# Attention by head pairs and query parts, the last queries of two heads in one tile, and the first MLP begun inside the first batch

## The chip, the cores and the metric

The kernel runs on one core of a Trainium2 chip. The metric is the device time of one execution in microseconds; the smaller the better. The core has TensorE (matmuls and transposes into the PSUM banks), VectorE, ScalarE, GpSimd and SyncE, each with its own queue of instructions worked off in order; they wait for each other by semaphores. In the profile they are PE (PEld for the loads of its stationary operand), DVE, ACT, POOL and SP.

## The reference

Three stages, all in float32 with an accuracy that the kernel reaches by splitting each matmul operand in a high and a low part and taking three products (or two, where one side needs no low part).

```python
def _attn_ref(q, k, v, s):                     # 4 batches, 8 heads, 576 tokens, 64 per head
    scores = scale * np.matmul(q, k.transpose(0, 1, 3, 2))
    cum = np.cumsum(np.maximum(s, 0.0), axis=-1)
    bias = -(cum[:, :, :, None] - cum[:, :, None, :])
    scores = np.where(causal, -1000000000.0, scores + np.minimum(bias, 0.0))
    attn = np.exp(scores - np.max(scores, axis=-1, keepdims=True))
    attn = attn / (np.sum(attn, axis=-1, keepdims=True) + 1e-09)
    return np.matmul(attn, v)

def _moe_ref(x, w_in, w_out, g_ln):            # 2304 tokens, 512 -> 1024 -> 512
    h = x @ w_in
    solu = h * softmax(h)
    ln = (solu - mean) / np.sqrt(var + 1e-06) * g_ln
    return ln @ w_out

def _moe2_ref(x, w_in, w_out):                 # 512 -> 2048 -> 512
    h = x @ w_in
    return (h * np.clip(h + 3.0, 0.0, 6.0) / 6.0) @ w_out
```

## The kernel before

One loop over slots `n` is written out for every engine; all engines run through the same slots and meet by counting semaphores. A head has five slots (`SLOTS`), one for each tile of 128 queries; the fifth tile has 64 (`TAIL`). In slot `k` of head `m` TensorE transposes the block row `k` of head `m`'s exponentials (`transpose_probs`, L488), and computes scores of head `m + 1` (`scores`, L474 to L478): four to five slots ahead of their transposes. VectorE adds the bias and takes the row maximum (`row_max`, L678), ScalarE the exponential and its row sum (`exp_row`, L835). The transposed block is copied by ScalarE as its high part (`copy_probs`, L846) and subtracted by VectorE for the low one (`split_probs`, L689). `weighted_values` (L507) multiplies with v for the queries of `CUTS`: the first 256 and the other 320; hi and lo of v stand side by side, so a product comes in two halves of partitions that `copy_corr` (ScalarE, L854) and `add_parts` (VectorE, L705) add into `xT`. For a pair of heads `scales` (L522) transposes the widened reciprocals of the sums and `scale_pair` (L713) multiplies.

SyncE loads q and k of a head together (each half of the 128 partitions gets the same 64 rows), its bias row and v. ScalarE rounds q and k (`split_qk`, L827), GpSimd subtracts the low part of q in the upper 64 partitions (L385) and of k (L387), splits v (L395, L397), widens the reciprocals (L402) and splits `w_in` in 16 parts (L409, L411).

The first MLP works on 18 tiles of 128 tokens (`t`), ten slots each (`TILE_SLOTS`), from slot `MOE_FROM` = 45 on, behind nine heads. Of a tile, `hidden` (L538) takes six slots, four matmuls each; then VectorE takes the maximum (`max1`), ScalarE the exponential (`exp1`, L871), VectorE the normalised product (`solu`, L729 to L737), ScalarE the square (`square`), GpSimd the reciprocal root, VectorE `norm` (L742). In the next tile's slots come the transposes (`transpose_ln`, L553) with copy and split, and `project` (L572): the tile pair's projection to 256 tokens, two of the four column blocks a tile, into one PSUM bank that ScalarE empties (`copy_x2`, L889). Two buffers `es` hold the exponentials of two tiles. From tile 12 (`ALONE`) there is no attention left, and hidden tiles take turns in two pairs of banks.

The attention of a batch must be complete before a token tile that lies in it is read: `split_x` waits for `x_done`. SyncE loads the first six chunks of the second MLP's weights when attention has ended, GpSimd splits them in the last five tiles' slots (`split_early`), and the second MLP follows, six groups of three token tiles, 16 chunks each (`hidden2`, L592 to L594, and `output`, L609 to L611). The order on TensorE is this loop:

```python
for n in range(-SLOTS, MOE_TO):
    m, k = n // SLOTS, n % SLOTS
    t, r = (n - MOE_FROM) // TILE_SLOTS, (n - MOE_FROM) % TILE_SLOTS
```

## Time and profile before

| | |
|---|---|
| device time, median of 2 runs | 961.86 us (961.58 to 962.13) |
| the profiled execution | 965.07 us, its span 963.0 us |
| TensorE busy | 866.0 us, 90% of the span |
| VectorE, ScalarE, GpSimd busy | 425.9, 435.1, 253.5 us |
| mean granted clock of TensorE | 0.958 of full speed |
| DMA | 51.38 MB |

The span goes from the first to the last instruction of the profile; the device time has about 2 us more. Busy is the time in which at least one instruction of the engine runs; a matmul's end is modelled, and matmuls overlap, so their mean length is more than the distance between their starts. Full speed of TensorE is 2.4 GHz, the other level 1.2 GHz.

### The profile page before, as it was taken

The page shows a single profiled execution, that of the slowest core. Times are in us where ns is not written, and L with a number is a line of the kernel's source. Part 1 is how long each engine was busy: PE and PEld are TensorE (multiplying, and loading weights), DVE is VectorE, ACT ScalarE, POOL GpSimd, SP SyncE. Part 2 cuts the span into 40 slices and gives each one's busy share as a digit, 9 for nine tenths or more (in the row PEclk, how much of TensorE's full clock was granted, in tenths as well). Part 3 has the DMA queues.
Part 4 walks back from the last instruction along what each step waited for, and adds up shares of the span by engine and source line. Part 5 has one row for each costly group of instructions (what it writes and reads, how often), then busy time and mean ns, then how long its engine had stood idle before and what let it go on. Part 6 is the DMA issues. An engine that isn't in the chain of part 4 may idle for free.

```text
span 963.0 us, 13828 instructions
## 1 busy us (share of the span) xinstructions
PE 866.0 (90%) x5008; PEld 765.0 (79%) x5008; DVE 425.9 (44%) x1037; ACT 435.1 (45%) x985; POOL 253.5 (26%) x291
## 2 busy tenths in 40 slices
PE   4588868988889989888988999999999999999997
PEld 3467647777777877776877999999999999999996
DVE  3466565666666666664434412233222222232222
ACT  4577665666666676663323335322222222222222
POOL 4477433443433443421364025100000000000000
PEclk9788778799999999999999999999999999999999
DMA  6554313313223322203000203000000000000000
GB/s 153 171 173 122 99 44 87 82 49 87 68 62 88 86 62 69 54 16 132 1 1 1 88 19 114 1 33 0 28 6 1 33 1 1 34 1 1 33 1 34
DMA packets 25779, 51.38 MB, mean 53 GB/s; under 512 B 5424, under 2 KB 9520, under 8 KB 25712
## 3 DMA queue, kind: packets, MB, share of 16 engines
q1 hardware_dynamic: 25712, 50.50, 18.3%
q8 instruction: 41, 0.67, 0.3%
q14 instruction: 26, 0.21, 0.1%
HBM read 45.69 MB, written 4.79 MB: 52 GB/s over the span
## 4 chain that ended last, share of the span: by engine, by line
PE 65%; ACT 12%; DVE 9%; issue 6%; POOL 4%; DMA 3%; SPq 1%; ACTq 0%; DVEq 0%; POOLq 0%
PE psum L538 9%; PE psum L594 7%; PE psum L592 7%; PE psum L610 7%; PE psum L593 7%; PE psum L611 7%; PE psum L609 7%; PE psum L572 4%; PE psum L507 4%; ACT prob L835 4%; PE psum L488 3%; DVE es L733 2%; ACT psum L877 2%; ACT qk_st L827 2%; DVE nmax L724 2%
## 5 line engine op out<-in xcount | busy, mean ns | idle before, releaser
L791 DVE SCALAR_TENSOR_TENSOR act<-act,psum 128x384 f32<-128x384 f32 x96 | 53.2, 554 | 292.0 <-ACT act L939 292.0
L939 ACT ACTIVATE act<-psum,three 128x384 f32<-128x384 f32 x96 | 55.8, 581 | 274.8 <-PE psum L594 274.8
L594 PE MATMUL psum<-x_hi,w_lo 128*128 128x384 f32 x384 | 129.5, 337 | 0.0
L592 PE MATMUL psum<-x_hi,w_hi 128*128 128x384 f32 x384 | 129.4, 337 | 0.0
L593 PE MATMUL psum<-x_lo,w_hi 128*128 128x384 f32 x384 | 129.0, 336 | 0.0
L835 ACT ACTIVATE prob<-prob,nmax 128x128 f32<-128x128 f32 (+4 forms) x160 | 95.8, 601 | 56.1 <-DVE nmax L678 55.2
L611 PE MATMUL psum<-w_hi,g_lo 128*128 128x512 f32 x288 | 113.9, 395 | 0.0
L610 PE MATMUL psum<-w_lo,g_hi 128*128 128x512 f32 x288 | 113.7, 395 | 0.0
L609 PE MATMUL psum<-w_hi,g_hi 128*128 128x512 f32 x288 | 112.0, 389 | 0.0
L488 PE MATMUL psum<-ident,prob 128*128 128x128 f32 (+1 forms) x480 | 78.6, 275 | 34.7 <-DVE pB_lo L689 16.9
L488 PEld LDWEIGHTS psum<-ident,prob 128*128 128x128 f32 (+1 forms) x480 | 54.1, 147 | 54.9 <-issue 38.4
L474 PE MATMUL psum<-qk_st 128*128 128x128 f32 (+2 forms) x192 | 76.7, 404 | 20.1 <-POOL k_lo L387 12.8
L572 PE MATMUL psum<-lnT_hi,w_out_hi 128*128 128x256 f32 x288 | 82.2, 286 | 13.6 <-ACT xT L889 13.4
L678 DVE CUSTOM_DVE_ANT_0 prob<-psum,bias 128x128 f32<-128x128 f32 (+4 forms) x160 | 83.2, 535 | 10.8 <-DMA bias<-cum_dram 8.3
L572 PE MATMUL psum<-lnT_lo,w_out_hi 128*128 128x256 f32 x288 | 82.1, 285 | 0.0
L572 PE MATMUL psum<-lnT_hi,w_out_lo 128*128 128x256 f32 x288 | 81.6, 283 | 0.0
L478 PE MATMUL psum<-k_lo,qk_st 128*128 128x128 f32 (+2 forms) x192 | 78.3, 408 | 0.0
L592 PEld LDWEIGHTS psum<-x_hi,w_hi 128*128 128x128 f32 x384 | 72.2, 188 | 4.1
L593 PEld LDWEIGHTS psum<-x_lo,w_hi 128*128 128x128 f32 x384 | 72.1, 188 | 4.0
L538 PE MATMUL psum<-w_in_hi,xs_hi 128*128 128x512 f32 x144 | 62.3, 432 | 12.9 <-POOL xs_lo L422 12.9
L594 PEld LDWEIGHTS psum<-x_hi,w_lo 128*128 128x128 f32 x384 | 72.0, 188 | 0.0
L689 DVE TENSOR_TENSOR pB_lo<-psum,pB_hi 128x384 fp32r<-128x384 f32 (+2 forms) x96 | 55.4, 577 | 33.9 <-ACT pB_hi L846 33.9
(92 smaller groups left out, 1834.4 us busy)
## 6 DMA issues: line engine op xcount, KB each, us to landing
qk_raw<-qkT SPq DMA_DIRECT2D x64, 288.0 KB, 4.2
bias<-cum_dram SPq DMA_DIRECT2D x32, 288.0 KB, 4.0
out<-out_sb SPq DMA_DIRECT2D x6, 768.0 KB, 3.5
v_raw<-v_main SPq DMA_DIRECT2D x32, 128.0 KB, 3.5
w_raw<-w_in SPq DMA_DIRECT2D x16, 256.0 KB, 3.3
w_raw<-w_out SPq DMA_DIRECT2D x16, 256.0 KB, 3.9
w_in_raw<-w_in SPq DMA_DIRECT2D x1, 2048.0 KB, 9.4
w_out_raw<-w_out SPq DMA_DIRECT2D x1, 2048.0 KB, 9.8
```

The costliest lines, as they stand in the source:

```text
L478: last = pe.matmul(ps, q, k_lo[p][:, lo_:hi_], start=False, stop=True)
L488: last = pe.transpose(ps[:, j * w:(j + 1) * w], prob[0:w, src:src + P], ident[0:w, 0:w])
L538: last = pe.matmul(bank(h_bank(t) + half), x, w, start=(n % 12 == 0), stop=(n % 12 == 11))
L572: last = pe.matmul(bank(project_bank(q), PJW), w, x, start=(n == 0), stop=(n == 23))
L592: pe.matmul(ps, w2_hi[f][:, cols], xh, start=(c_ == 0), stop=False)
L593: pe.matmul(ps, w2_hi[f][:, cols], xl, start=False, stop=False)
L594: last = pe.matmul(ps, w2_lo[f][:, cols], xh, start=False, stop=(c_ == NC - 1))
L609: pe.matmul(bank(4 + k), gh, w2_hi[f][:, NC * P:], start=(f == 0), stop=False)
L610: pe.matmul(bank(4 + k), gh, w2_lo[f][:, NC * P:], start=False, stop=False)
L611: last = pe.matmul(bank(4 + k), gl, w2_hi[f][:, NC * P:], start=False, stop=(f == NF2 - 1))
L678: dve.tensor_tensor_reduce(out=prob[0:rows, BLK[i] * P:BLK[i] * P + n], in0=psum[0:rows, at:at + n], in1=bias[p][0:rows, 0:n], scale=-SCAL ...
L835: sc.activation(tile, tile, ACT.Exp, scale=-1.0, bias=nmax[0:rows, p, i:i + 1], accum_out=rsum[0:rows, p, i:i + 1]).then_inc(exp_done, 1)
```

## The change

**Units.** A unit is a head pair and a part of the queries. The first kind has the first 256 queries (tiles 0 and 1), two items: item `k` has both tiles of head `k`. The second kind has the other 320, five items: tile 2 and tile 3 of head 0, the same of head 1, and as fifth item the last 64 queries of both heads in one tile of 128 rows. For that tile q of one head stands in columns 0 to 63 and of the other in 64 to 127, with zeros in the rest, and the scores of both heads are added in one bank. A batch is four units of the first kind and then four of the second: 28 items, 112 in all, instead of 160 slots. q and k of a head are loaded and split twice, for its first unit (256 and 256 columns) and for its second (384 and 576), into three buffers; v too (two blocks, then five). The sums of a pair are scaled once a unit.

**Distance.** Scores run two items ahead of their transposes, in three banks; the fifth block of an item 4 is transposed into a free piece of bank 2, and the scores of a later item that need the bank of an item 4 wait for that item's `split_probs`.

**The first MLP** begins at item 14. A tile `t` has six steps, laid on the items `STARTS[t]` to `STARTS[t + 1]`, 9, 9, then 7 and 6 items long; 14 tiles begin and the loop ends at item 134. Hidden and projection matmuls stand ahead of and behind the scores of the item. There is one buffer `es`, one pair of hidden banks (but for tile 16) and one bank for projections and the transposes of the MLP. `split_x`'s high part and `copy_x2` move from ScalarE to VectorE, where `max1` and `solu` stand ahead of the item's row maximum. `w_in` is loaded in four DMAs from item 0 on and split from item 3 on, `w_out` is split at items 24 to 31. The early chunks of the second MLP load behind the last scaling and are split at items 120 to 131.

```diff
+PAIRS = HEADS // 2
+UNITS = BATCH * 2 * PAIRS
+FIRST_KIND = [u % (2 * PAIRS) < PAIRS for u in range(UNITS)]
+BASE = [0]
+for _kind in FIRST_KIND:
+    BASE.append(BASE[-1] + (2 if _kind else 5))
+ITEMS = BASE[UNITS]
+ITEM = [(u, k) for u in range(UNITS) for k in range(BASE[u + 1] - BASE[u])]
+TILES = [((0, k, k), (1, k, 2 + k)) if FIRST_KIND[u] else
+         ((2 + k % 2, k // 2, 2 * (k % 2) + k // 2),) if k < 4 else ((4, None, 4),) for u, k in ITEM]
+TILES_BEFORE = [0]
+LOS_BEFORE = [0]
+for _tiles in TILES:
+    TILES_BEFORE.append(TILES_BEFORE[-1] + len(_tiles))
+    LOS_BEFORE.append(LOS_BEFORE[-1] + (2 if _tiles[0][0] == NQ - 1 else 1))
+S_BANKS = [((2 * (u % PAIRS) + k) % 3,) if FIRST_KIND[u] else ((0,), (1,), (2,), (0,), (1, 2))[k] for u, k in ITEM]
+S_BEFORE = [max([m for m in range(n) if set(S_BANKS[m]) & set(S_BANKS[n])], default=-1) for n in range(ITEMS)]
+TAIL_AT = 2 * BANK - 288
...
+STARTS = [14, 23] + [32 + 7 * i for i in range(4)] + [60 + 6 * i for i in range(8)] + [109, 116, 122, 128, 134]
+STEPS = 6
+END = STARTS[NT]
+STEP_AT = {}
+for _t in range(NT):
+    for _r in range(STEPS):
+        STEP_AT[STARTS[_t] + _r * (STARTS[_t + 1] - STARTS[_t]) // STEPS] = (_t, _r)
+FIRST_STEP = STARTS[0]
 W_IN_PARTS = 16
+W_IN_FROM, W_OUT_FROM, EARLY_FROM = 3, 24, 120
...
+def sums_slot(u, e):
+    return BASE[u + 1] + (1 if FIRST_KIND[u] else e)
+def scales_slot(u):
+    return BASE[u + 1] + 2
...
+SPLIT_AT = {}
+for _u in range(UNITS):
+    SPLIT_AT.setdefault(BASE[_u] - 3, []).append((_u, 0))
+    SPLIT_AT.setdefault(BASE[_u] - (2 if FIRST_KIND[_u] and _u % (2 * PAIRS) else 1 if _u else 2), []).append((_u, 1))
+VALUES_SLOT = {}
+VALUES_AT = {}
+for _u in range(UNITS):
+    for _e in range(2):
+        VALUES_SLOT[_u, _e] = BASE[_u] + (1 + _e if not FIRST_KIND[_u] else _e)
+        VALUES_AT.setdefault(VALUES_SLOT[_u, _e], []).append((_u, _e))
+X_AT = {STARTS[t] - 2: t for t in range(NT)}
...
-        es = [sb(first, f"es{p}", [P, F1]) for p in range(2)]
+        es = sb(first, "es", [P, F1])
...
+            def scores(n):
+                u, k = ITEM[n]
+                c = kind(u)
+                last_load = load_of(u, 1 if k == 4 else TILES[n][0][1])
+                pe.wait_ge(q_lo_done, last_load + 1)
+                pe.wait_ge(k_lo_done, last_load + 1)
+                if S_BEFORE[n] >= 0:
+                    pe.wait_ge(max_done, TILES_BEFORE[S_BEFORE[n] + 1])
+                    if ITEM[S_BEFORE[n]][1] == 4:
+                        pe.wait_ge(pT_lo_done, LOS_BEFORE[S_BEFORE[n] + 1])
+                    elif 2 in S_BANKS[n] and any(ITEM[m][1] == 4 for m in range(max(0, n - 5), n)):
+                        m = max(m for m in range(n) if ITEM[m][1] == 4)
+                        pe.wait_ge(pT_lo_done, LOS_BEFORE[m + 1])
+                for tile, e, _ in TILES[n]:
+                    at, w = scores_of(n, tile), KW[tile]
+                    q_at = (tile if c else tile - 2) * P
+                    diag0 = tile * P
+                    heads = (0, 1) if e is None else (e,)
+                    for lo_, hi_ in [(0, w)] if w <= BANK else [(0, w // 2), (w // 2, w)]:
                         ps = psum[:, at + lo_:at + hi_]
-                        pe.matmul(ps, q, k_hi[:, lo_:hi_], start=True, stop=False)
-                        if hi_ > diag0:
-                            pe.matmul(psum[:, at + diag0:at + hi_], ident_bf[:, :], mask_bf[:, 0:hi_ - diag0],
-                                      start=False, stop=False)
-                        last = pe.matmul(ps, q, k_lo[p][:, lo_:hi_], start=False, stop=True)
+                        for e_ in heads:
+                            p = load_of(u, e_) % 3
+                            q = qk_hi[p][:, q_at:q_at + P]
+                            keys = slice(QW[c] + lo_, QW[c] + hi_)
+                            pe.matmul(ps, q, qk_hi[p][:, keys], start=(e_ == heads[0]), stop=False)
+                            if hi_ > diag0 and e_ == heads[0]:
+                                mask = mask_tail if e is None else mask_bf
+                                pe.matmul(psum[:, at + diag0:at + hi_], ident_bf[:, :], mask[:, 0:hi_ - diag0],
+                                          start=False, stop=False)
+                            last = pe.matmul(ps, q, qk_lo[p][:, keys], start=False, stop=(e_ == heads[-1]))
                 last.then_inc(scores_ready, 1)
 
-            def transpose_probs(m, i):
-                pe.wait_ge(exp_done, NQ * m + i + 1)
-                n = SLOTS * m + i
-                wait(pe, pT_lo_done, n if n >= MOE_FROM else n - 1)
-                ps, w = bank(turn(m, i)), ROWS[i]
-                for j in range(i + 1):
-                    src = (BLK[i] + j) * P
-                    last = pe.transpose(ps[:, j * w:(j + 1) * w], prob[0:w, src:src + P], ident[0:w, 0:w])
...
+            def transpose_probs(n):
+                pe.wait_ge(exp_done, TILES_BEFORE[n + 1])
+                before = n - 2 if n <= FIRST_STEP else n - 1
+                if before >= 0:
+                    pe.wait_ge(pT_lo_done, LOS_BEFORE[before + 1])
+                ps = bank(turn(n))
+                j = 0
+                for tile, _, _ in TILES[n]:
+                    for b in range(tile + 1):
+                        src = prob_of(n, tile) + b * P
+                        dst = psum[:, FIFTH:FIFTH + P] if b == NQ - 1 else ps[:, j * P:(j + 1) * P]
+                        last = pe.transpose(dst, prob[:, src:src + P], ident[:, :])
+                        j += 1
                 last.then_inc(pT_ready, 1)
 
-            def weighted_values(h, c):
-                pe.wait_ge(v_lo_done, h + 1)
-                pe.wait_ge(pT_lo_done, NQ * h + (2, NQ)[c])
-                if c == 1:
-                    pe.wait_ge(sum_done, 2 * h + 1)
-                elif h % 2 == 0:
...
+            for n in range(-2, END):
+                t, r = STEP_AT.get(n, (None, None))
+                if n in SCALES_AT:
+                    scales(SCALES_AT[n])
+                for u, e in SUMS_AT.get(n, ()):
+                    weighted_values(u, e)
+                if 0 <= n < ITEMS:
+                    transpose_probs(n)
+                if r in (1, 2) and t >= 1:
+                    transpose_ln(t - 1, r - 1)
+                if r in (0, 1, 2):
+                    hidden(t, 8 * r, 8 * r + (8, 4, 4)[r])
+                if r in (3, 4, 5) and t >= 2:
+                    q = 2 * (t - 2) + (r - 3) // 2
+                    project(q, (0, 16, 8)[r - 3], (8, 24, 16)[r - 3])
+                if 0 <= n + 2 < ITEMS:
+                    scores(n + 2)
+                if r in (1, 2):
+                    hidden(t, 8 * r + 4, 8 * r + 8)
+                if r in (3, 4, 5) and t >= 2:
+                    q = 2 * (t - 2) + (r - 2) // 2
+                    project(q, (8, 0, 16)[r - 3], (16, 8, 24)[r - 3])
 
             for g in range(NG):
...
+            def split_x(t):
+                dve.wait_ge(x_done, units_before(t))
+                wait(dve, h_ready, t)
+                dve.tensor_copy(xs_hi[:, :, :], xT[:, :, t * P:(t + 1) * P]).then_inc(xs_hi_done, 1)
...
+            def copy_x2(q):
+                g, d = q // NC, q % NC
+                dve.wait_ge(x2_ready, q + 1)
+                dve.tensor_copy(xT[:, d, PJW * g:PJW * (g + 1)], bank(L_BANK, PJW)).then_inc(x2_done, 1)
...
+            for n in range(-2, END + 1):
+                t, r = STEP_AT.get(n, (None, None))
+                if r == 0 and t >= 3:
+                    copy_x2(2 * (t - 3) + 1)
+                if r == 3:
+                    max1(t)
+                if r == 4:
+                    solu(t)
+                if 0 <= n + 1 < ITEMS:
+                    for tile, e, col in TILES[n + 1]:
+                        row_max(n + 1, tile, e, col)
+                for u, e in SUMS_AT.get(n, ()):
+                    add_parts(u, e)
+                if 0 <= n < ITEMS:
+                    split_probs(n)
+                for u in range(UNITS):
+                    if BASE[u + 1] == n:
+                        invert(u)
+                if n in SCALES_AT:
+                    scale_pair(SCALES_AT[n])
+                if n in X_AT:
+                    split_x(X_AT[n])
+                if r == 0 and t >= 1:
+                    norm(t - 1)
+                if r in (1, 2) and t >= 1:
+                    split_ln(t - 1, r - 1)
+                if r == 4 and t >= 2:
+                    copy_x2(2 * (t - 2))
+                if W_OUT_FROM <= n < W_OUT_FROM + NF1:
+                    split_w_out(n - W_OUT_FROM)
+                if t == NT - 1 and r in (1, 2, 4, 5):
+                    split_x2(0, (1, 2, 4, 5).index(r))
+            norm(NT - 1)
+            copy_x2(NPJ - NC - 1)
...
+            behind = consts_done, 4
+            w_in_next = 0
+            for n in range(-3, END + 1):
+                t, r = STEP_AT.get(n, (None, None))
+                if n + 1 in STARTS[:NT]:
+                    behind = split_x(STARTS.index(n + 1))
+                if r == 5:
+                    behind = variance(t)
+                for u in range(UNITS):
+                    if BASE[u + 1] == n:
+                        behind = widen(u)
+                for u, e in VALUES_AT.get(n, ()):
+                    behind = split_v(u, e)
+                for u, e in SPLIT_AT.get(n, ()):
+                    behind = split_qk(u, e, behind)
+                for _ in range(1 if n < 8 else 2):
+                    if n >= W_IN_FROM and w_in_next < W_IN_PARTS:
+                        behind = split_w_in(w_in_next)
+                        w_in_next += 1
+                if n >= EARLY_FROM and n - EARLY_FROM < 2 * EARLY:
+                    split_early(n - EARLY_FROM)
...
+            for n in range(-3, END):
+                t, r = STEP_AT.get(n, (None, None))
+                sums = n in SUMS_AT
+                if 0 <= n < ITEMS and not sums:
+                    copy_probs(n)
+                if 0 <= n + 1 < ITEMS:
+                    for i, (tile, e, col) in enumerate(TILES[n + 1]):
+                        exp_row(n + 1, i, tile, col)
+                for u, e in SUMS_AT.get(n, ()):
+                    copy_corr(u, e)
+                if 0 <= n < ITEMS and sums:
+                    copy_probs(n)
+                if r in (1, 2) and t >= 1:
+                    copy_ln(t - 1, r - 1)
+                if r == 3:
+                    exp1(t)
+                if r == 4:
+                    square(t)
+                if W_OUT_FROM <= n < W_OUT_FROM + NF1:
+                    split_w_out(n - W_OUT_FROM)
+                if t == NT - 1 and r in (1, 2, 4, 5):
+                    split_x2(0, (1, 2, 4, 5).index(r))
+                for u, e in SPLIT_AT.get(n, ()):
+                    split_qk(u, e)
...
+    tails = np.zeros((NH, DH, P), np.float32)
+    tails[0::2, :, :TAIL] = qT[0::2, :, cut:]
+    tails[1::2, :, P - TAIL:] = qT[1::2, :, cut:]
     arrays = {
-        "qkT": np.stack([x.reshape(NH, SEQ, DH).transpose(0, 2, 1) for x in (q, k)], axis=2),
-        "v_main": v[:, :cut].reshape(NH, NQ - 1, P, DH).transpose(0, 2, 1, 3).reshape(NH, P, (NQ - 1) * DH),
+        "qk0": np.concatenate([qT[:, :, :CUT], kT[:, :, :CUT]], axis=2),
+        "qk1": np.concatenate([qT[:, :, CUT:cut], tails, kT], axis=2),
+        "v_main": v[:, :cut].reshape(NH, NQ - 1, P, DH).transpose(0, 2, 1, 3),
         "v_tail": v[:, cut:],
         "s": s.reshape(NH, SEQ),
```

`hidden`, `project`, `max1`, `exp1`, `solu`, `square`, `variance`, `norm`, `copy_ln`, `split_ln` and the second MLP keep their arithmetic.

## Rows read from the trace of the kernel before

**Rows 1.** Table of windows: stretch, its length, busy us (instructions) by engine, clock, DMA
```profile
...
0.00:113.00 113.00, 76.89 (x452) 65.41 (x453) 60.45 (x194) 70.37 (x177) 67.14 (x95) 0.84 0.53 147
113.00:189.00 76.00, 61.48 (x314) 50.01 (x315) 48.42 (x123) 46.60 (x108) 28.70 (x31) 0.77 0.25 65
189.00:441.50 252.50, 225.56 (x1574) 195.40 (x1573) 160.49 (x432) 162.65 (x397) 97.18 (x111) 1.00 0.24 65
441.50:543.50 102.00, 87.55 (x551) 77.79 (x552) 42.60 (x68) 32.47 (x64) 35.75 (x42) 0.97 0.14 46
543.50:963.00 419.50, 414.55 (x2122) 376.34 (x2121) 113.91 (x221) 123.04 (x244) 24.70 (x12) 1.00 0.06 21
```

**Rows 2.** Timeline of TensorE: starts of five hidden tiles (start us, us, instruction)
```profile
...
113.00 0.77 PE L538 MATMUL psum<-w_in_hi,xs_hi 128*128 128x512 f32 x1 [0.30 <-POOL xs_lo L422]
...
206.32 0.47 PE L538 MATMUL psum<-w_in_hi,xs_hi 128*128 128x512 f32 x1
...
433.48 0.47 PE L538 MATMUL psum<-w_in_hi,xs_hi 128*128 128x512 f32 x1
...
455.14 0.50 PE L538 MATMUL psum<-w_in_hi,xs_hi 128*128 128x512 f32 x1 [1.33 <-POOL xs_lo L422]
...
529.26 0.50 PE L538 MATMUL psum<-w_in_hi,xs_hi 128*128 128x512 f32 x1 [2.10 <-POOL xs_lo L422]
```

**Rows 3.** List of waits of TensorE over the span
```profile
...
PE psum L488 <- DVE pB_lo L689: 16.9, 18, 4.0
PE psum L488 <- ACT prob L835: 16.2, 22, 2.0
PE psum L572 <- ACT xT L889: 13.4, 10, 2.4
```

**Rows 4.** Groups of instructions by form, GpSimd: count, busy us, mean ns, idle before
```profile
...
L387 POOL TENSOR_TENSOR k_lo<-qk_raw,qk_st 128x576 fp32r<-128x576 f32 x32 | 45.6, 1426 | 2.5
...
L397 POOL TENSOR_TENSOR v_sp<-v_raw,v_sp 128x320 fp32r<-128x320 f32 x32 | 27.9, 872 | 2.6
...
L395 POOL CAST v_sp<-v_raw 128x320 fp32r<-128x320 f32 x32 | 19.0, 595 | 0.0
...
L411 POOL TENSOR_TENSOR w_in_lo<-w_in_raw,w_in_hi 128x256 fp32r<-128x256 f32 x16 | 11.7, 731 | 1.3
...
L409 POOL CAST w_in_hi<-w_in_raw 128x256 fp32r<-128x256 f32 x16 | 6.3, 397 | 10.5 <-DMA w_in_raw<-w_in 10.5
```

**Rows 5.** The same view, VectorE and ScalarE on attention's blocks
```profile
...
L689 DVE TENSOR_TENSOR pB_lo<-psum,pB_hi 128x512 fp32r<-128x512 f32 x32 | 22.0, 687 | 10.5 <-ACT pB_hi L846 10.5
...
L846 ACT ACTIVATE pB_hi<-psum 128x512 fp32r<-128x512 f32 x32 | 18.8, 588 | 1.0 <-PE psum L488 1.0
```

**Rows 6.** Timeline from 396.8 to 401.6 us
```profile
...
396.84 0.36 PE L572 MATMUL psum<-lnT_hi,w_out_hi 128*128 128x256 f32 x1 [1.22 <-ACT xT L889]
...
397.87 0.60 PE L488 MATMUL psum<-ident,prob 128*128 128x128 f32 x4
397.98 0.14 DVE L729 TENSOR_SCALAR den<-esum 128x1 f32<-128x1 f32 x1
...
398.22 0.47 PE L474 MATMUL psum<-qk_st 128*128 128x512 f32 x1
...
399.68 0.15 DVE L737 TENSOR_SCALAR neg_mu<-solu_sum 128x1 f32<-128x1 f32 x1
...
401.12 0.49 PE L488 MATMUL psum<-ident,prob 64*128 64x64 f32 x5 [0.66 <-ACT prob L835]
```

**Rows 7.** Timeline from 136.9 to 142.2 us
```profile
...
136.90 0.75 DVE L717 SCALAR_TENSOR_TENSOR w_out_lo<-w_out_raw,g_sb,w_out_hi 128x512 fp32r<-128x512 f32 x1 [1.88 <-ACT w_out_hi L860]
...
140.17 1.42 POOL L385 TENSOR_TENSOR qk_st<-qk_raw,qk_st 64x576 fp32r<-64x576 f32 x1 [4.74 <-ACT qk_st L827]
...
140.76 1.37 DVE L717 SCALAR_TENSOR_TENSOR w_out_lo<-w_out_raw,g_sb,w_out_hi 128x512 fp32r<-128x512 f32 x1
```

**Rows 8.** Timeline at 301.8 us, SyncE
```profile
...
301.78 1.10 SPq L304 DMA_DIRECT2D qk_raw<-qkT  x2
```

738 lines of the change are left out of this document (365 added, 373 removed).

## The prediction

> **What bounds the kernel now.** I read the table of windows first [rows 1]. From 543.5 us on TensorE is busy 414.6 of 419.5 us: the second MLP is TensorE's own work, and the change leaves it alone. From 189.0 to 441.5, where attention and the first MLP run together, TensorE is busy 225.6 of 252.5 at the full clock: it is the bound there too, but 11% goes in waits. After the last attention (441.5 to 543.5) it is busy 87.6 of 102.0. The first two windows are the weak ones: busy 76.9 of 113.0 at a granted clock of 0.84, then 61.5 of 76.0 at 0.77, where busy time is partly stretched by the 1.2 GHz level. The first MLP's first matmul starts at 113.0 [rows 2], since its loop begins behind nine heads. The list of waits [rows 3] says what TensorE stands for: the split of the transposed block before (16.9 us), the exponential (16.2) and the copy of a projected bank (13.4).
>
> Next, what TensorE needs. Hidden tiles start 28.4 us apart in the steady window (206.3 to 433.5 is eight periods) [rows 2]; so it holds 8.9 tiles and 17.8 heads, and a period of two heads and a tile has 25.3 us busy [rows 1]. Some three waits per period each leave about 0.2 us of a modelled matmul tail in that, so I take 24.8. In the window without attention a tile's period is 14.8 us (455.1 to 529.3 is five) [rows 2], its busy part 12.7, its need 12.4. That leaves 6.2 us a head. By this count 54 us are lost before 113.0 (9.3 heads, 58 of need), about 28 from 113.0 to 189.0 (no projections yet), 31.5 in the steady window (3.5 a tile) and 16.5 after it. These 130 us are what the change can win from.
>
> **The last queries of two heads in one tile.** Per pair of heads ten transposes of 64 rows become five of 128. Four of 128 took from 397.87 to 398.22, 0.088 each; five of 64 were busy 0.49, so at most 0.098 each and by the spacing of the others about 0.08 [rows 6]. So 80 of 480 transposes go at 0.086: **7 us** less for TensorE. The score matmuls keep their columns (eight of 288 per pair), the values' too. VectorE and ScalarE lose 16 row maxima and exponentials and some small splits, but VectorE gains two narrow multiplications a pair, and two copies moved from ScalarE: the first half of a token tile's split (18) and the projected banks (36). With row maxima and splits at 0.3 to 0.7 us, as the split of [rows 5], I count 13.7 us of attention a pair on VectorE and 7.5 us a tile, so about 75 to 80% of a steady step against 64% now [rows 1]. Not yet bound, but fuller.
>
> **The start.** By the diff the MLP begins at item 14: four light units (2 items each) and the first items of two heavy ones. TensorE needs 23 us for this. I price GpSimd's queue, for it holds most there. A column of the low parts costs 1.426/576 = 2.5 ns [rows 4], and 64 rows cost as much as 128 [rows 7]. Eight light loads of 2x256 columns: 10.1 us. Four heavy ones of 384+576: 9.5. Values: ten splits, eight of them of 128 instead of 320 columns (1.47 for 320, 0.65 taken for 128): 8.1. W_in in 16 parts of 0.40+0.73: 18.0 [rows 4]. Widening and the first token tile: 3.6. Together 49 us. The first values land near 14.5 us (the bias needs the same two DMA trips as now, with SyncE's issues ahead), and about 4 us of the 49 lie before. So 14.5+45, and 2 for gaps: **hidden starts at 62 us** (bounds 55, if queues overlap better, and 75, if each item waits for ScalarE's split as well). The 10.5 us that GpSimd waits for w_in's single DMA [rows 4] go, since it comes in four and is used by quarters. Lost before hidden: 62-23 = 39 against 54, **-15**. If w_in were not behind everything else here, the items' own chain of about 2.2 us each would give 45: this is the cover under which the extra loading of q, k and v in two units a head (half as many columns again) is free.
>
> **Items 14 to 31**, with hidden tiles 0 and 1 and no projection. A step with hidden work has 3.6 us for TensorE, one without is held at about 2.3 by transposes, copy, exponential and the next split of q and k. The step behind the softmax of the MLP waits for VectorE (below), 4.8. Two tiles come to 57, and w_out's splits, which now fall in here, add some 4: 61, of which 44 is need. Lost 17 against 28: **-11** (bounds -20 and 0; at a clock of 0.77, as in [rows 1], it would be near 0).
>
> **The steady part**, 80 items, 12.5 tiles. The ring that now takes 16.9 us [rows 3] is transposes, copy (0.59), split (0.69) [rows 5], next transposes; 1.7 us with the semaphores. Now some 2.5 us of other matmuls stand beside it, after the change 3.4. That helps. Three things speak against. Scores run two items ahead instead of four to five slots, so a late row maximum reaches the next transposes. In the loop of VectorE the MLP's maximum and its normalising product come before the row maximum and the split; the product with its small operations takes 1.85 us (397.98 to 399.83) [rows 6]. And the projected bank is copied by VectorE behind all of these. I follow one such step: its TensorE part reaches the second projection after 2.5 us; the product starts 0.8 us into the step, for it waits for ScalarE's exponential, then come 1.9, row maximum 0.6, split 0.6, copy 0.35: the bank is free after 4.3. So **1.8 us** a tile against the 1.2 seen at 396.84 [rows 6]. The fifth item of a heavy unit makes the scores two items on wait for its own splits (the fifth block lies in a score bank): 2.2 us with 1 to 2 of cover, 0.6 a tile. Jitter and steps without MLP work 0.6. Sum 3.0 a tile, 37 us lost, against 31.5 now, over 12.5 tiles instead of 8.9: **+6**. Bounds 1.8 a tile (only the bank; 22 us) and 5 (62).
>
> One contention shows here. The second half of w_out's split, VectorE with two operands in SBUF, took 0.75 us with GpSimd idle and 1.37 while GpSimd's 1.42 us subtraction ran, ending 0.54 behind it [rows 7]. The Trainium skill, page "SBUF — State Buffer", section "Who interferes with whom", has it as a lock, and says that a plain copy from SBUF to SBUF may hold it too. The trace agrees for the two-operand form; no row has VectorE's copy. If it holds for the 18 moved copies, each would stand up to 1.4 us, 18 x 0.7 = 13 us on VectorE and, a third of it exposed, 4 more on the end. I leave this out of the sum.
>
> **Alone.** Attention now ends with 6.9 periods of MLP to go, after the change with 3.3 to 3.5. A period there loses 2.4 now; with one buffer for the exponentials and one bank pair for most tiles hidden must wait for the square, but the projections (5.9 us) stand beside that chain of about 6.2. I take 2 to 2.5 a tile: 8 against 16.5, **-8** (bounds -10 and 0). SyncE issues 20 loads a pair of heads instead of 10, 0.55 us each [rows 8]: 11 us in the 28 of a steady pair, and in the 15 to 25 of one at the start: hidden, at nothing; without that cover a unit's second load would come some 2 us late. The early weights of the second MLP load after item 114 and are split in 12 steps of some 2 us within 50 us: hidden too.
>
> **Sum**, against the profiled span of 963.0: -7 -15 -11 +6 -8 = -35, so 928. The profiled execution took 965.07, the median of the two timed is 961.86, 0.33% below; its span is 0.1% above that median. I forecast 927 for the median, 3.6% faster. A measurement here tells about 2% from no change: 942.6 and 981.1 are the marks.
>
> **Rivals.** (a) *The waits are covered.* With 3.4 us of matmuls beside each ring the losses of the steady part fall to 1.8 a tile (-15) and the start is bound by the items' chain (-7): 905. For it: VectorE is idle a third of the steady window. Against: order in the queue, not load, makes these waits. Chance 0.24. (b) *VectorE's order takes the gain back.* If the product and the maximum each hold up two items' row maxima a tile, 5 us a tile are lost: +25, 952, within 2%. For it: TensorE waits for exponentials today [rows 3], although its scores run far ahead. Chance 0.19. (c) *Two items of lead are too few*, and it gets slower: every item runs the chain transposes, copy, exponential, with VectorE's MLP share between, 4.8 us instead of 4.0 over 98 items: +78, 1006. It decides from 0.55 us an item (981). Against: row maxima need only scores issued an item before, and nothing else is in front in four of six steps. Chance 0.09. (d) *The early start buys nothing*, since GpSimd holds the items to 75 us or more and the clock stays at the 1.2 GHz level to 120: -7+6-8 and +0 from the start, 954. Chance 0.06. The forecast itself, 912 to 942: 0.42.
>
> Faster than 942.6 is forecast and (a), 0.66 with a little of (b) counted; within 2% 0.23; slower 0.11. Range 898 to 958: it takes in (b) and (d) and most of (a).
>
> **What would show it.** Transposes 400 from attention instead of 480. First hidden matmul near 62 us, GpSimd over 75% busy before it. First matmul of the second MLP near 508, and 419 from there to the end. Projection waits for VectorE's copy, 1.8 us each, at the head of TensorE's waits. The granted clock 1.00 from item 32 on. Wrong would be a first hidden matmul behind 75, or more than 5 us of idle time a tile from item 32 to 111.

## The result, and the profile after

The changed kernel takes 982.95 us (981.87 to 984.03, median of 2) against 961.86: 1.022 of the time before, with an interval of 1.017 to 1.027. It is slower by 2.2% (1.7 to 2.7); 3.6% faster was forecast. Its profiled span is 980.1 us, at a mean clock of 0.956. TensorE is busy 868.6 us of it, VectorE 432.1, ScalarE 409.5, GpSimd 309.0.

The table of windows, cut where the stages change: the first hidden matmul (67.0), item 32 (145.2), the last item (502.0), the second MLP (557.0). The columns are those of [rows 1].

```profile
0.00:67.00 67.00, 42.63 (x189) 34.25 (x189) 29.56 (x94) 34.67 (x89) 51.14 (x94) 0.92 0.60 163
67.00:145.20 78.20, 54.44 (x293) 45.10 (x294) 43.70 (x117) 43.97 (x101) 36.17 (x51) 0.80 0.45 122
145.20:502.00 356.80, 308.52 (x2010) 272.16 (x2008) 215.96 (x570) 194.18 (x447) 166.71 (x230) 0.95 0.36 92
502.00:557.00 55.00, 46.86 (x306) 42.56 (x305) 26.11 (x55) 15.91 (x28) 31.03 (x36) 0.97 0.29 96
557.00:980.10 423.10, 416.10 (x2122) 377.91 (x2120) 116.78 (x225) 120.81 (x236) 23.97 (x10) 1.00 0.06 19
```

To compare these with [rows 1] I price TensorE's work by the spacing of its starts at the full clock in the trace of before, each kind of matmul by itself, and call the rest of a stretch lost. Before: 54.7 us lost to 113.0, then 28.3, 32.0, 17.2, and 5 in the second MLP. After: 43.2 to the first hidden matmul, 34.7 from there to item 32, 65.8 in the 80 items, 9.7 alone, and the second MLP 3.6 us longer. In all TensorE has 8.5 us less work (817 for 826) and loses 26 us more (163 for 137). The 80 items have more than all of that: 5.3 us a tile (65.8 over 12.5) for 3.6 before (32.0 over 8.9); the other stretches together lose less than before. In these items the clock falls too: 36.4 us lie at 1.2 GHz, which costs about 17.5 of the 65.8 (busy time, 308.5, less the work at the full clock, 291); the other 48.3 are idle time. Before, the window from 189 to 441.5 had none at 1.2 GHz.

The list of waits of TensorE, its head (waited-for, us, times, longest):

```profile
PE psum L663 <- issue: 29.4, 22, 4.2
PE psum L766 <- DVE xT L966: 20.4, 13, 3.3
PE psum L663 <- POOL qk_lo L550: 20.4, 5, 6.8
PE psum L663 <- DVE p_lo L884: 12.3, 10, 2.3
PE psum L663 <- POOL qk_hi L547: 7.9, 5, 2.4
...
PE psum L682 <- ACT prob L1057: 2.4, 2, 1.5
```

The waits that led before are gone or small: for the exponential 2.4 (16.2 in [rows 3]), and the split is hardly a wait of the transposes any more (2.0) but one of the scores. In their place stand q and k of the next unit (`qk_hi`, `qk_lo`: 28.3), the "issue" of the scores, the bank of the projection, copied by VectorE (20.4), and the split of the fifth item (12.3). All but the bank are waits of `scores` (L663), which now run only two items ahead. "Issue" names no releaser; `scores` waits there for q and k, for row maxima and for the split, and e3 below shows how much of it hangs on q and k.

The 28.3 us for q and k lie mostly in front of the 80 items: 10.4 before 67.0, 10.9 from there to item 32, 7.1 in the 80 items. Of the scores' "issue" 15.3, of the bank 13.1 and of the split 8.1 us lie in the 80 items.

One stretch of the timeline shows how they come about:

```profile
306.15 0.48 PE L668 MATMUL psum<-qk_lo,qk_hi 128*128 128x512 f32 x1
...
307.58 1.23 DVE L935 TENSOR_REDUCE nmax<-psum 128x1 f32<-128x1024 f32 x1 [0.88 <-PE psum L737]
...
308.72 0.68 DVE L875 CUSTOM_DVE_ANT_0 prob<-psum,bias 128x512 f32<-128x512 f32 x1
...
310.17 0.42 PE L668 MATMUL psum<-qk_lo,qk_hi 128*128 128x384 f32 x1
...
310.75 0.48 DVE L904 TENSOR_TENSOR xT<-psum,xT 64x320 f32<-64x320 f32 x1 [1.34 <-ACT xT L1088]
...
311.13 1.11 ACT L1099 ACTIVATE es<-psum,nmax 128x1024 f32<-128x1024 f32 x1
...
312.75 1.28 DVE L944 SCALAR_TENSOR_TENSOR es<-psum,rden,es 128x1024 f32<-128x1024 f32 x1
...
314.23 0.56 DVE L875 CUSTOM_DVE_ANT_0 prob<-psum,bias 128x384 f32<-128x384 f32 x1
...
314.83 0.61 ACT L1057 ACTIVATE prob<-prob,nmax 128x384 f32<-128x384 f32 x1 [2.50 <-DVE nmax L875]
...
316.64 0.69 DVE L884 TENSOR_TENSOR p_lo<-psum,p_hi 128x512 fp32r<-128x512 f32 x1
...
317.58 0.42 DVE L966 COPY xT<-psum 128x256 f32<-128x256 f32 x1
...
318.14 0.55 PE L766 MATMUL psum<-lnT_hi,w_out_hi 128*128 128x256 f32 x1 [3.26 <-DVE xT L966]
```

The scores of an item of 512 keys have been issued at 306.15, and VectorE is free from 306.70. But its next instruction is the MLP's maximum (L935), which waits 0.88 us for TensorE's hidden tile to end and then takes 1.23; the row maximum behind it starts at 308.72. The next scores, issued at 310.17, meet the same. VectorE has the rest of its item to do, for which it waits 1.34 us for ScalarE (310.75), and is through with it at 312.1. Then it waits for ScalarE's exponential of the MLP (311.13) and makes the product (312.75), and the row maximum starts at 314.23, over 3.5 us after the scores; some 2 us of that are the MLP's share. ScalarE stood 2.50 us for it (314.83); its copy of the transposes, the split (316.64) and the copy of the projected bank (317.58) all follow late, and TensorE stands 3.26 us at 318.14. Behind this wait the clock falls to 1.2 GHz.

The change itself made this order. In the kernel before, VectorE's loop had row maximum and split in front (L764, L766) and the MLP's maximum and product behind them (L781, L783).

### The profile page after: what moved, and what is told of

It is laid out like the page before. It is cut to its first block, busy times and chain, and to the rows that moved or that the text cites. A ratio compares the mean times of both kernels' runs of the same rounds, so it can differ in the third digit from the quotient of the medians.

```text
span 980.1 us, 13896 instructions
## 1 busy us (share of the span) xinstructions
PE 868.6 (89%) x4912; PEld 772.0 (79%) x4912; DVE 432.1 (44%) x1059; ACT 409.5 (42%) x901; POOL 309.0 (32%) x419
## 4 chain that ended last, share of the span: by engine, by line
PE 74%; DVE 8%; issue 6%; ACT 6%; POOL 4%; DMA 1%; SPq 1%; ACTq 0%; DVEq 0%; POOLq 0%
PE psum L737 10%; PE psum L766 7%; PE psum L788 7%; PE psum L786 7%; PE psum L787 7%; PE psum L804 7%; PE psum L805 7%; PE psum L803 7%; PE psum L707 5%; PE psum L682 3%; PE psum L663 3%; PE psum L668 2%; DVE es L944 2%; ACT es L1099 2%; PE psum L750 1%
## 5 line engine op out<-in xcount | busy, mean ns | idle before, releaser
L663 PE MATMUL psum<-qk_hi 128*128 128x128 f32 (+2 forms) x192 | 70.0, 370 | 70.0 <-issue 29.4
L1057 ACT ACTIVATE prob<-prob,nmax 128x128 f32<-128x128 f32 (+4 forms) x144 | 83.6, 581 | 113.1 <-DVE nmax L875 112.9
L547 POOL TENSOR_TENSOR qk_hi<-qk_raw,qk_hi 64x256 fp32r<-64x256 f32 (+1 forms) x64 | 55.9, 873 | 169.2 <-ACT qk_hi L1049 167.7
L663 PEld LDWEIGHTS psum<-qk_hi 128*128 128x128 f32 x192 | 40.3, 210 | 85.2 <-issue 57.7
L766 PE MATMUL psum<-lnT_hi,w_out_hi 128*128 128x256 f32 x288 | 86.9, 302 | 20.4 <-DVE xT L966 20.4
L1080 ACT ACTIVATE p_hi<-psum 128x512 fp32r<-128x512 f32 (+2 forms) x128 | 62.6, 502 | 93.5 <-PE psum L682 92.0
L884 DVE TENSOR_TENSOR p_lo<-psum,p_hi 128x512 fp32r<-128x512 f32 (+2 forms) x128 | 71.9, 572 | 45.2 <-ACT p_hi L1080 43.0
L766 PE MATMUL psum<-lnT_hi,w_out_lo 128*128 128x256 f32 x288 | 86.0, 299 | 0.0
L766 PE MATMUL psum<-lnT_lo,w_out_hi 128*128 128x256 f32 x288 | 85.7, 298 | 0.0
L682 PE MATMUL psum<-ident,prob 128*128 128x128 f32 x400 | 74.2, 310 | 4.7 <-ACT prob L1057 2.4
L875 DVE CUSTOM_DVE_ANT_0 prob<-psum,bias 128x128 f32<-128x128 f32 (+3 forms) x128 | 59.9, 487 | 38.5 <-PE psum L668 33.6
L766 PEld LDWEIGHTS psum<-lnT_hi,w_out_hi 128*128 128x128 f32 x288 | 58.2, 202 | 23.5 <-issue 23.2
L668 PE MATMUL psum<-qk_lo,qk_hi 128*128 128x128 f32 (+2 forms) x192 | 76.0, 401 | 0.0
```

The costliest lines, as they stand in the source:

```text
L663: pe.matmul(ps, q, qk_hi[p][:, keys], start=(e_ == heads[0]), stop=False)
L668: last = pe.matmul(ps, q, qk_lo[p][:, keys], start=False, stop=(e_ == heads[-1]))
L682: last = pe.transpose(dst, prob[:, src:src + P], ident[:, :])
L766: last = pe.matmul(bank(L_BANK, PJW), w, x, start=(n == 0), stop=(n == 23))
L1057: sc.activation(p, p, ACT.Exp, scale=-1.0, bias=nmax[:, u % 2, col:col + 1], accum_out=rsum[:, u % 2, col:col + 1]).then_inc(exp_done, 1)
```

## The experiments

Three theories. T1: TensorE waits because VectorE's queue holds ready row maxima behind the MLP's maximum and product, which wait for others (rival (b) of the prediction). T2: three smaller choices, none of them the units themselves, make the waits of the scores and of the bank: a wait wider than needed, a copy moved to a fuller queue, q and k rounded last. T3: the units are at fault: loading twice, or two items of lead, or the early start. Spans are of one profiled execution each; ratios are medians against the kernel before on the same chip. The experiments ran on four chips, so where two versions differ little the ratios tell more than the times.

### Three single edits on the changed kernel

**e1_bank1_free.** The fifth item's fifth block lies in score bank 2. The wait of `scores` for its split is kept only where bank 2 is reused.

```diff
-                    if ITEM[S_BEFORE[n]][1] == 4:
+                    if ITEM[S_BEFORE[n]][1] == 4 and 2 in S_BANKS[n]:
```

> The changed kernel with one wait less: the scores of a heavy unit's second item, which lie in bank 1 alone, no longer wait for the split of the fifth item's transposed blocks (whose fifth block lies in bank 2). If each wait on TensorE in the changed trace is a loss of its own, the 12.3 us that scores wait for that split (10 times) go, and a little half-clock time behind them: a span of 965 to 970 instead of 980. If the real limit is who feeds the scores two items ahead (q and k splits), the same steps wait for something else instead: 976 or more.

Measured: 974.93 us, ratio 1.013 (1.010 to 1.016), span 974.4. Waits of TensorE, two of the list:

```profile
PE psum L766 <- DVE xT L966: 25.0, 15, 3.0
PE psum L663 <- POOL qk_hi L547: 20.6, 8, 6.1
```

The wait for `p_lo`, 12.3, left the head of the list, and 5.7 us came of it. The bank went from 20.4 to 25.0 and `qk_hi` from 7.9 to 20.6, while `qk_lo` went from 20.4 to 8.2: the same late chain was met at the next place. The span lies between the two ranges that were expected.

**e2_x2_on_scalar.** `copy_x2` goes back to ScalarE, behind `copy_probs`.

```diff
-                dve.tensor_copy(xT[:, d, PJW * g:PJW * (g + 1)], bank(L_BANK, PJW)).then_inc(x2_done, 1)
+                sc.activation(xT[:, d, PJW * g:PJW * (g + 1)], bank(L_BANK, PJW), ACT.Copy).then_inc(x2_done, 1)
```

> The changed kernel with the copies of the projected banks back on ScalarE, right behind the item's block copy, instead of VectorE behind product, row maximum and split. If VectorE's order is what projections wait for (20.4 us, 13 times, up to 3.3 each, with a fall to the 1.2 GHz level behind the longest), the wait falls under 8 us and the span to 955 to 965. If the copy's place is a symptom of steps that are late anyway, TensorE waits for exponentials or row maxima instead, and the span stays above 974.

Measured: 973.56 us, ratio 1.011 (1.008 to 1.015), span 972.6:

```profile
PE psum L663 <- issue: 38.0, 25, 4.2
...
PE psum L766 <- ACT xT L1105: 5.2, 6, 2.1
```

The wait for the bank fell from 20.4 to 5.2, and the scores' "issue" grew from 29.4 to 38.0: half was given back. This too is between the two expected ranges.

**e3_split_first.** ScalarE rounds q and k at the head of an item in place of its end.

```diff
                 sums = n in SUMS_AT
+                for u, e in SPLIT_AT.get(n, ()):
+                    split_qk(u, e)
                 if 0 <= n < ITEMS and not sums:
```

> The changed kernel with ScalarE's rounding of q and k as the first operation of its item instead of the last. If scores starve because GpSimd gets the rounded q and k a step late (scores wait 28 us for GpSimd's subtractions and another 29 us at the same matmul with no releaser named), these waits halve and the span is 945 to 960. If instead the loads themselves or GpSimd's own queue are late, ScalarE only stands idle at the head of its step, in front of the block copy, and the span is 980 or more.

Measured: 969.82 us, ratio 1.007 (1.004 to 1.011), span 970.6:

```profile
PE psum L766 <- DVE xT L966: 29.4, 14, 2.9
PE psum L663 <- DVE p_lo L884: 26.6, 12, 4.8
...
PE psum L663 <- issue: 7.9, 6, 3.1
PE psum L663 <- POOL qk_lo L550: 7.0, 1, 7.0
...
PE psum L663 <- POOL qk_hi L547: 3.5, 2, 2.2
```

`qk_hi` fell from 7.9 to 3.5, `qk_lo` from 20.4 to 7.0 and the scores' "issue" from 29.4 to 7.9, together from 57.7 to 18.4. So most of this "issue" hangs on q and k too: the place of the rounding on ScalarE made the largest group of waits. But the bank rose to 29.4 and `p_lo` to 26.6, and the span fell by 9.5 us where 20 or more were expected.

**e4_all_three.** The three together.

> The three edits together. If they are separate losses the gains add: 12 + 20 + 25, a span near 925 to 935, faster than the kernel before. If they share one chain (an item's length set by the longest of several rings), less than two thirds of the sum comes: 945 to 960.

Measured: 944.34 us, ratio 0.982 (0.979 to 0.985), span 941.4:

```profile
PE psum L707 <- issue: 13.5, 11, 3.5
PE psum L663 <- issue: 13.0, 10, 4.3
PE psum L682 <- ACT prob L1045: 9.7, 8, 3.7
```

This is 38.7 us under the changed kernel's span, where the single edits sum to 22.7. One late chain is seen at several points; each edit alone moves the wait to the next. Of the 57 us that were expected for separate losses two thirds came, but of what the single edits gave 1.7 times. T2 holds, as far as it goes. That the changed kernel with three small edits beats the one before also speaks against T3.

### What is left, from the version with all three

**f1_transposes_twice.** The fifth items' transposes are issued twice, 80 in all: the price of what merging the last queries removes.

```diff
-                        last = pe.transpose(dst, prob[:, src:src + P], ident[:, :])
+                        for _ in range(2 if ITEM[n][1] == 4 else 1):
+                            last = pe.transpose(dst, prob[:, src:src + P], ident[:, :])
```

> The version with all three edits, and every transpose of a fifth item issued twice (the same data to the same place), which puts back as many 128-row transposes as the merged last queries save (80). If TensorE's own work sets the end, the prediction's term returns: 80 x 0.086 = 7 us, a span of 947 to 949 against 941.4. If the merged tile's work lies beside waits, 2 us or less.

Measured: 949.51 us, ratio 0.984 (0.980 to 0.989), span 943.7, 2.3 over e4. The median is 5.2 over e4's, but on another chip; the ratios differ by 0.003 (2.5 us) and their intervals overlap. It is repeated on the best version below.

**f2_late_start.** The first MLP begins at item 32, the start of the second batch, with 12 tiles beside attention and 6 alone.

```diff
-STARTS = [14, 23] + [32 + 7 * i for i in range(4)] + [60 + 6 * i for i in range(8)] + [109, 116, 122, 128, 134]
+STARTS = [32 + 7 * i for i in range(12)] + [116 + 6 * i for i in range(7)]
-W_IN_FROM, W_OUT_FROM, EARLY_FROM = 3, 24, 120
+W_IN_FROM, W_OUT_FROM, EARLY_FROM = 3, 24, 134
```

> The version with all three edits, but the first MLP begins at item 32 instead of 14 (tiles 7 items long for the first twelve, then 6; it ends at item 152, the early weights' splits moved to item 134). The prediction credited the early start with 11 us for items 14 to 31 and 8 for the shorter end, of the 15 before item 14 nothing changes here: if that holds, a span near 960. The rival is that losses only move: without the MLP items 14 to 31 take about 2.4 us each, and what is lost at the end comes back there: 938 to 948.

Measured: 970.57 us, ratio 1.006 (1.003 to 1.008), span 968.5, that is 27.1 more than e4. Its first hidden matmul comes at 130.5, its second MLP at 545.4. In the version with all three edits the early start is worth 27 us, more than either expectation had. They do not lie where the prediction put them. By the pricing of the work above, 4 of them are lost before item 32 and 21 in the 80 items behind it (59.9 lost against 39.2, and 37 us at 1.2 GHz against 15); the end, with six tiles alone, loses hardly more than e4's.

**f3_row_max_first.** On VectorE the row maximum of the next item stands ahead of the MLP's maximum and product.

```diff
+                if 0 <= n + 1 < ITEMS:
+                    for tile, e, col in TILES[n + 1]:
+                        row_max(n + 1, tile, e, col)
                 if r == 3:
                     max1(t)
                 if r == 4:
                     solu(t)
-                if 0 <= n + 1 < ITEMS:
-                    for tile, e, col in TILES[n + 1]:
-                        row_max(n + 1, tile, e, col)
```

> The version with all three edits, and on VectorE the row maximum of the next item ahead of the MLP's maximum and product instead of behind. If the product in front of the row maximum is what exponentials and transposes wait for (9.7 us, 8 times), the span falls by 5 to 10, to 931 to 936. The rival: the product then waits for the row maximum, the square and the next hidden tile come later, and nothing is won: 939 to 944.

Measured: 920.0 us, ratio 0.954 (0.950 to 0.958), span 918.0, 23.4 under e4, more than twice what was expected. It is the best version, 4.6% faster than the kernel before. Its table of windows:

```profile
67.30:137.30 70.00, 50.62 (x294) 41.78 (x294) 43.31 (x117) 44.09 (x101) 37.26 (x52) 0.90 0.51 136
137.30:443.00 305.70, 290.89 (x2008) 257.93 (x2007) 204.76 (x546) 200.78 (x470) 166.13 (x229) 0.99 0.41 107
443.00:494.80 51.80, 46.13 (x307) 41.11 (x305) 25.28 (x48) 18.71 (x36) 31.26 (x36) 1.00 0.30 97
494.80:918.00 423.20, 416.18 (x2120) 377.97 (x2120) 113.93 (x221) 122.43 (x240) 23.99 (x10) 0.99 0.06 20
```

The 80 items and the end of the last take 305.7 us where the changed kernel took 356.8, and the clock is 0.99 where it was 0.95.

**f4_qk_before_v.** GpSimd takes q and k ahead of the widening and the values.

```diff
+                for u, e in SPLIT_AT.get(n, ()):
+                    behind = split_qk(u, e, behind)
                 for u in range(UNITS):
...
-                for u, e in SPLIT_AT.get(n, ()):
-                    behind = split_qk(u, e, behind)
```

> The version with all three edits, and on GpSimd the split of q and k ahead of widening and of the values' split. If GpSimd's own order still delays scores (6.3 and 6.8 us named, 13.0 with no releaser), the span falls by 4 to 10. The rival: GpSimd stands waiting for ScalarE's rounding while the values' split is ready, values come later, and it is the same or slower: 941 to 948.

Measured: 942.46 us, ratio 0.978 (0.973 to 0.982), span 943.3 against e4's 941.4: nothing. GpSimd's own order is not the limit in this version.

### How much the order is by itself

**g1_order_alone.** The edit of f3 alone, on the changed kernel.

> The changed kernel with VectorE's order alone turned (row maximum ahead of the MLP's maximum and product), nothing else. If this order is the one cause, it alone brings the 23 us that it brought on top of the three other edits, or more: a span of 950 to 957. If the scores' other waits (q and k late, the fifth item's bank, the projected bank) bind as well, the row maximum only waits for scores instead: 965 to 975.

Measured: 952.17 us, ratio 0.986 (0.984 to 0.988), span 950.2: 29.9 us under the changed kernel. The waits of VectorE and ScalarE, first in the changed kernel:

```profile
ACT prob L1057 <- DVE nmax L875: 112.9, 62, 5.2
...
DVE nmax L935 <- PE psum L737: 14.9, 16, 3.4
```

then in g1:

```profile
ACT prob L1057 <- DVE nmax L875: 74.2, 48, 5.2
...
DVE nmax L935 <- PE psum L737: 2.1, 6, 0.5
```

VectorE stood 14.9 us in 16 waits for a hidden tile to end, and 2.1 with the row maximum in front; ScalarE's exponentials wait 38.7 us less for row maxima. On TensorE the bank falls from 20.4 to 13.2, but the scores wait as before:

```profile
PE psum L663 <- issue: 27.1, 24, 3.8
PE psum L663 <- POOL qk_lo L550: 20.1, 5, 6.9
PE psum L766 <- DVE xT L966: 13.2, 12, 2.4
```

T1 is shown: this one edit gives more than the other three give singly in sum, and turns 2.2% slower into 1.4% faster. It does not remove the scores' waits for q and k.

**g2_order_bank_split.** The best version with `copy_x2` on VectorE again (the edit of e2 taken back).

> Order, bank and ScalarE's split first, but the projected banks' copies left on VectorE: the best version less one edit. With the order turned the copy still stands behind row maximum, product and the item's split, so the prediction's step (bank free 4.3 us into the item, TensorE there after 2.5) holds: 10 to 20 us slower than 918. If with everything else on time the copy is on time as well: 918 to 924.

Measured: 935.85 us, ratio 0.970 (0.968 to 0.972), span 933.6, 15.6 over the best. One of TensorE's waits:

```profile
PE psum L766 <- DVE xT L966: 23.0, 15, 2.4
```

The moved copy costs 15.6 us here and 7.5 where other waits hid it. The 15 waits are 1.5 us each in the mean, and 15.7 us, 1.3 a tile, lie in the 80 items, where the prediction worked out 1.8.

**g3_softmax_last.** Version e4 with the MLP's maximum and product moved behind the split, the other end of the order.

```diff
-                if r == 3:
-                    max1(t)
-                if r == 4:
-                    solu(t)
                 if 0 <= n + 1 < ITEMS:
...
                     split_probs(n)
+                if r == 3:
+                    max1(t)
+                if r == 4:
+                    solu(t)
```

> The best version with the MLP's maximum and product moved further back on VectorE, behind the item's sums and split too. If the ring of transposes, copy and split is still exposed in those items, 3 to 8 us faster: 910 to 915. If the MLP's own chain (exponential, product, square, next hidden tile) is now the later one, slower: 920 to 930.

Measured: 946.97 us, ratio 0.981 (0.979 to 0.984), span 944.7, 26.7 over the best. TensorE then waits 10.8 us for exponentials, 9.4 for the bank and 9.5 for `qk_hi`. Both expected ranges, 910 to 915 and 920 to 930, were missed; it is even slower than e4, though it is much the order that the kernel before had. The sums and the split wait for ScalarE in their turn and hold up the MLP's chain: ScalarE's exponential of the MLP waits 32.6 us for the maximum, 7.9 in the best version. Of the three orders tried, the one with only the row maximum in front is the best.

**h1_twice_on_best.** The edit of f1 on the best version.

> The best version (span 918.0), with the transposes of every fifth item issued twice, as in the earlier run on a version that waited more. There 80 transposes cost 2.3 us of span, a third of what the prediction has. If the rest was hidden beside waits, it costs more here, where few waits are left: 5 to 7 us, a span of 923 to 925. If a repeated transpose is simply cheap, 2 to 3 us again: 920 to 921.

Measured: 920.38 us, ratio 0.953 (0.950 to 0.955), span 918.8 against 918.0. Its timeline on TensorE:

```profile
293.24 1.25 PE L683 MATMUL psum<-ident,prob 128*128 128x128 f32 x10
294.33 0.60 PE L751 MATMUL psum<-ident,es 128*128 128x128 f32 x4
```

Ten transposes take 1.09 us of starts, 0.109 each, so 80 more are 8.7 us of TensorE's time; 0.8 shows in the span, and nothing in the ratio (0.953 for 0.954). That is less than both expectations.

## Why the prediction was wrong

**Steady part: the step that failed.** The prediction lost 3.0 us a tile in the 80 items (1.8 the bank, 0.6 the fifth item's bank, 0.6 jitter), 37 us in all. Measured were 65.8, 5.3 a tile. It followed one item in which the product stands before the row maximum, but charged this order to the projected bank alone; and it had no wait of the scores for q and k and no time at the lower clock. The table has TensorE from item 32's transposes to those of item 111, in us; "lost" is by the pricing of the work above:

| | changed kernel | e3 | g1 | best (f3) |
|---|---|---|---|---|
| scores for q and k, or "issue" | 22.4 | 2.2 | 19.6 | 6.0 |
| projected bank | 13.1 | 22.0 | 5.9 | 1.8 |
| split of the transposes | 9.8 | 15.2 | 6.4 | 1.2 |
| idle in all | 48.3 | 42.7 | 32.5 | 14.8 |
| at 1.2 GHz | 36.9 | 34.5 | 15.4 | 7.3 |
| lost | 66.6 | 57.4 | 39.9 | 15.7 |

The order on VectorE alone (g1) is worth 26.7 of the 29 us that the forecast missed here: 15.8 of idle time and, for the rest, less time at 1.2 GHz. The bank itself took 1.0 us a tile and not 1.8, and the scores' wait for the fifth item's split (8.1) is the 0.6 that was said. That g1's 39.9 comes near the forecast's 37 is in part luck: the bank has 5.9 for 22, and the scores' 19.6 stood at nothing. These 19.6 do not come from late row maxima, for they stay when the order is turned. They come from ScalarE's rounding of q and k at the end of its item: in e3 they are 2.2. The prediction's "nothing else is in front in four of six steps" looked at VectorE alone. The order is rival (b): it put "+25" on it, and g1 gives 26.7, so mechanism and price were right; its time, 952, fell short of 980 by the misses outside it. With the three smaller edits and the old order (e4) 39.2 us are lost.

**The clock.** "The granted clock 1.00 from item 32 on" was wrong: 36.4 us were at 1.2 GHz, 17.5 us lost. It fell nine times between item 32 and the last item, each time behind a wait of TensorE of 1.3 to 3.3 us, as at 318.14, and with most waits gone it is 0.99. That the waits set it off is the reading of these windows; no run held the waits and changed the clock.

**Items 14 to 31.** The prediction had 17 us lost, a gain of 11, with 0 as the bound at a clock of 0.77. Measured were 34.7 lost, 6.4 more than before, which is outside that bound, at a mean clock of 0.80 with 31.9 us at 1.2 GHz. Idle were 23.8 us, 16.8 of them scores that waited for q and k or with no releaser named; the lower clock makes the rest. The term had both at nothing. e4 and f3 have a clock of 0.84 and 0.90 there.

**Start.** First hidden matmul at 67.0 us for 62 (bounds 55 and 75); lost 43.2 for 39. GpSimd is busy 51.1 of the 67.0 us, 76%, for the 49 that were summed, as the pricing of its queue foretold. That it is the limit there is argued from this, not shown; no edit moved the first hidden matmul out of 66.2 to 67.4 but f2's. Of the 26 us that the terms of the start and of the items behind it promised, 5 came in the changed kernel (11.5 less 6.4). That f2 gives 27 against e4 is no proof of these terms: most of it lies in the 80 items.

**Merged transposes.** 400 for 480, as said. What goes is 160 of 64 rows, and 80 of 128 rows come. Five of 64 took 0.42 us up to the next matmul (median of 29 at the full clock before), five of 128 take 0.47 (median of 12 after), so the merge frees some 16 x 0.38 = 6 us of TensorE's time, near the 7. But the -7 was set on the path. 80 transposes more, 8.7 us, cost 0.8 and 2.3 us of span (h1, f1), so it is likely that most of what the merge frees goes into waits of the same items; no run undid the merge itself.

**Alone and second MLP.** 9.7 us lost for 8: right, and the sum's -8 held. The second MLP was forecast as unchanged and is 3.6 us longer: both halves of the MLP's transposes now share a bank (a wait of 1.89 us at 563.7 for the split of the first half); the other 1.7 us were not taken apart.

**Sum.** The misses against the terms are 4 (start), 18 (items 14 to 31), 29 (80 items), 2 (alone), 4 (second MLP): 57, for the 52 between 928 and 980.1. The other 5 go the other way: the forecast's 928 holds 822 of work, and TensorE had 817.

**Rivals.** (a) describes the steady part of the best version (15.7 lost, 1.3 a tile, for its 1.8), not this kernel. (c), two items of lead, is refuted as the cause: the best version has the same lead. Whether a longer lead would have covered the late row maxima was not tried. (d) does not fit: hidden began at 67.0 and not behind 75, and without the early start it is slower (f2). The price of loading q, k and v twice was not measured by itself; the best version pays it and is faster than the kernel before. Not settled is how the 62 us between the changed kernel and the best split between the edits: singly they give 5.7, 7.5, 9.5 and 29.9 (52.6), on top of others 15.6 for the bank and 23.4 for the order.

## What to carry to other kernels

When two streams of work share an engine's queue, list for each instruction what it waits for and what ready work stands behind it; load says nothing here (VectorE was 60% busy in the 80 items, and its order cost 30 us of the span). Put in front what is ready first and feeds the longest chain, and follow a late instruction on through every queue, not to the first waiter only. Waits on one chain replace each other, so a single edit that gives half of its wait back is no proof of a small cost: try the likely edits together before the change is given up. A wait with no releaser named is to be followed by an edit: here "issue" led to q and k. And work that leaves the busiest engine counts only where that engine does not wait in the same items anyway.

## What the hardware showed that was not expected

`norm` (VectorE, 128x1024, both sides in SBUF) kept its form and halved its time. Before, all its instructions by line (ns: least, median, most):

```profile
L742 DVE TENSOR_SCALAR es<-es,neg_mu,rstd x18: 812/1752/1772, 145.8 to 544.6; 128x1024 f32<-128x1024 f32 x18
```

and after:

```profile
L953 DVE TENSOR_SCALAR es<-es,neg_mu,rstd x18: 774/803/1326, 105.2 to 554.8; 128x1024 f32<-128x1024 f32 x18
```

Before, it started beside GpSimd's subtraction for the next token tile, as here:

```profile
403.52 1.29 POOL L422 TENSOR_TENSOR xs_lo<-xT,xs_hi 128x512 fp32r<-128x512 f32 x1
403.60 1.77 DVE L742 TENSOR_SCALAR es<-es,neg_mu,rstd 128x1024 f32<-128x1024 f32 x1
```

It ended 0.56 us behind GpSimd's end. After the change the two start several microseconds apart (for example 317.74 and 326.42), for the subtraction has moved to an earlier item. So some 15 us of VectorE's time (30.3 to 15.0) were this contention, and the change removed it by the way. The Trainium skill, "SBUF — State Buffer", "Who interferes with whom", has a lock between VectorE and GpSimd which this operation (`tensor_scalar`) can run into, and by which the later of the two stands until the first is done. The rows agree in kind: it is late when GpSimd is ahead of it. That it stood fully until GpSimd's end they do not show, for the 0.56 us behind that end are less than the 0.80 that it takes alone. The plain copies for which the prediction allowed 0.7 us each (`xs_hi`) took 0.46 in the mean, 0.40 at least and 0.62 at most: nearly nothing was lost there. But only two of the 18 ran for 0.3 us beside a subtraction that GpSimd had begun before, and these took 0.57 and 0.62.
